# First q and k by tiles, and the order of splits, clears and copies around it, in a one-core attention and mixture-of-experts kernel

## The reference

```
attention: q, k, v are (4, 8, 576, 64); window of 64 keys back, causal
    scores = q k^T / 8, masked; softmax; times v  -> x (2304, 512)
mixture of experts, E = 8, F = 1024:
    noisy = x @ w_gate + log1p(exp(x @ w_noise)) * noise
    the two largest of noisy per row choose two experts, softmax of the two gives their weights
    out[row] += weight * (relu(x[row] @ w1[e]) @ w2[e])
dense part, F2 = 2048:
    h = x @ w_in;  g = h * clip(h + 3, 0, 6) / 6;  out = g @ w_out
```

## Time and profile before

| | |
|---|---|
| median of 3 runs | 1018.13 us (1018.12 to 1018.77) |
| profiled execution, its own time | 1019.22 us |
| its span, first to last instruction | 1017.5 us |
| TensorE busy | 988.1 us, 97% |
| VectorE, ScalarE, GpSimd busy | 417.8, 227.7, 423.5 us |
| mean granted TensorE clock | 0.991 |

### The profile page before, as it was taken

The page is one execution under the profiler, slowest core; times in us unless marked ns, Lnnn a source line. Parts: engine busy times, 40 slices in busy tenths (PEclk is TensorE's granted clock), DMA queues, the critical chain, the costliest instruction groups (busy, mean ns, idle before and its releaser), DMA issues.

```text
span 1017.5 us, 18019 instructions
## 1 busy us (share of the span) xinstructions
PE 988.1 (97%) x7108; PEld 877.5 (86%) x7108; DVE 417.8 (41%) x897; ACT 227.7 (22%) x537; POOL 423.5 (42%) x326
## 2 busy tenths in 40 slices
PE   7989889999999999999999999999999999999998
PEld 6777668989889898989989989999999999999997
DVE  3578764313222222213222255545445445355333
ACT  4666521111111111111111121111111211111111
POOL 3067976993855739192855729101101001000000
PEclk9999879999999999999999999999999999999999
DMA  9699876764452716263342433200101111000000
GB/s 181 128 207 247 271 258 222 246 186 150 135 185 90 230 61 208 70 180 122 125 145 86 151 106 125 64 32 21 42 31 41 41 31 41 31 1 1 32 1 31
DMA packets 125878, 115.94 MB, mean 114 GB/s; under 512 B 64912, under 2 KB 93520, under 8 KB 125808
## 3 DMA queue, kind: packets, MB, share of 16 engines
q1 hardware_dynamic: 106368, 75.36, 27.0%
q10 hardware_dynamic: 13680, 20.75, 6.0%
q0 software_dynamic: 5760, 18.88, 5.8%
HBM read 75.90 MB, written 39.06 MB: 113 GB/s over the span
## 4 chain that ended last, share of the span: by engine, by line
PE 81%; SPq 7%; POOL 5%; DMA 3%; issue 2%; DVE 1%; ACT 0%; ACTq 0%; POOLq 0%; DVEq 0%
PE PS L1635 20%; PE PS L1755 20%; PE PS L1739 19%; PE PS L1618 19%; SPq L500 3%; SPq L490 3%; POOL x_sorted L711 3%; PE PS L1602 1%; POOL W L690 1%; POOL W L680 1%; PE PS L1680 1%; DMA x_sorted<-zeros 1%; DMA y_sorted<-y_sb 0%; PE PS L1498 0%; DMA stage<-in_moe_w_dram 0%
## 5 line engine op out<-in xcount | busy, mean ns | idle before, releaser
L1635 PE MATMUL PS<-W,hs_room 128*128 128x512 f32 (+1 forms) x960 | 245.2, 399 | 0.1
L1618 PEld LDWEIGHTS PS<-xs,W 128*128 128x128 f32 x1536 | 231.0, 189 | 10.8 <-issue 0.2
L1618 PE MATMUL PS<-xs,W 128*128 128x256 f32 (+2 forms) x1536 | 239.7, 307 | 0.0
L1755 PE MATMUL PS<-W,gs 128*128 128x512 f32 x864 | 217.0, 396 | 0.9 <-DVE gs L1353 0.9
L1739 PE MATMUL PS<-x2s,W 128*128 128x384 f32 x1152 | 216.6, 337 | 0.0
L1739 PEld LDWEIGHTS PS<-x2s,W 128*128 128x128 f32 x1152 | 201.4, 188 | 7.2
L680 POOL TENSOR_TENSOR W<-stage,ones_f 128x1024 fp32r<-128x1024 f32 (+1 forms) x100 | 147.6, 1484 | 136.5 <-PE PS L1635 133.1
L1635 PEld LDWEIGHTS PS<-W,hs_room 128*128 128x128 f32 (+1 forms) x960 | 172.3, 186 | 34.6 <-DVE hs_room L1203 0.3
L1755 PEld LDWEIGHTS PS<-W,gs 128*128 128x128 f32 x864 | 161.5, 188 | 31.5 <-issue 1.6
L690 POOL TENSOR_TENSOR W<-stage,W 128x1024 fp32r<-128x1024 f32 (+1 forms) x100 | 185.4, 1863 | 5.8
L1203 DVE SCALAR_TENSOR_TENSOR hs_room<-PS,hs_room 128x256 fp32r<-128x256 f32 (+2 forms) x128 | 61.9, 484 | 290.6 <-ACT hs_room L899 290.6
(11 more groups left out here) (133 smaller groups left out, 574.4 us busy)
## 6 DMA issues: line engine op xcount, KB each, us to landing
stage<-in_moe_w_dram SPq DMA_DIRECT2D x64, 512.0 KB, 4.2
x_sorted<-zeros SPq DMA_DIRECT2D x7, 1280.0 KB, 7.6
y_sorted<-y_sb ACTq DMA_DIRECT2D x33, 256.0 KB, 3.7
x_in<-x_sorted ACTq DMA_DIRECT2D x31, 256.0 KB, 4.3
vD<-in_v_dram SPq DMA_DIRECT2D x72, 64.0 KB, 2.8
out_dram<-o_sb SPq DMA_DIRECT2D x18, 256.0 KB, 2.1
stage<-in_moe_w_in_dram SPq DMA_DIRECT2D x8, 512.0 KB, 3.9
stage<-in_moe_w_out_dram SPq DMA_DIRECT2D x8, 512.0 KB, 3.8
```

Of the source, the lines that this page charges most:

```text
L1618: last = nc.tensor.matmul(HP_[:, c % 2, 0:n], W[:, par, 0, b, at:at + P], xs[part][:, a, kd, 0:n], start=start, stop=(kd == KD - 1 and (a, ...
L1635: last = nc.tensor.matmul(Y[0:n, first + t, :], hs[:, c % 2, a, t * P:t * P + n], W[:, par, 1, b, c * DM:(c + 1) * DM], start=(c == 0 and ...
L1755: last = nc.tensor.matmul(OP[:, tt, :], gs[:, c % 2, a, tt * P:(tt + 1) * P], W[:, 1, c // FC, b, at:at + DM], start=(c == 0 and (a, b) == ...
```

## The change

- Start. Item 0 is now tile 0 with all heads and item 1 tile 1 with all heads (`turn_tile`), so `scores(0)` runs before the transposes of tile 1. `transpose_p(0, 0)` comes before item 2, and item 2 is turned into two other PSUM banks, so it does not wait for `exps(0)`. v of tile 0 goes through ScalarE's queue, the gate weights through GpSimd's, v of tile 1 is issued before chunk 3.
- Chunks 4 and 8, which cross no batch, are loaded by four transfers and not six; `sem_inc` stands in for the missing counts.
- In iterations 5, 6, 7, 9, 10, 11, 13 and 14, at which a lot is routed, ScalarE copies k too (`move_both`, `chooses`).
- GpSimd no longer splits chunks 3 and 4 at tiles 12 and 13. Lots 0 and 1 are sent a little denser, chunk 3 is split between the eight transfers of lot 2, and chunks 4 and 5 after them. Chunks 6 and 7 are split by ScalarE (`beside_hi`) and VectorE (`beside_lo`) during expert 0.
- Weight chunk 7 is loaded at tile 17 and not 15, and three parts of `y_sorted` are cleared right behind it, where before one was cleared at 17 and two after the rows of expert 0 were there.
- The last lot is ranked behind `project` of chunk 1 and not behind `hidden` of chunk 3; `tables` and `places_in_y` come a chunk later.

```diff
-    FIRST_AT = (4, 6, 8, 10, 12, 13, 14, 15)
-    SPLIT_AT = (7, 8, 11, 12, 13)
+    FIRST_AT = (4, 6, 8, 10, 12, 13, 14, 17)
+    SPLIT_AT = (7, 8, 11)
+    BESIDE = 2
...
-    ZERO_AT = (16, 17)
+    ZERO_AT = (16, 17, 17, 17)
...
-    SCATTER_AT = {8: 0, 9: 1, 10: 2, 12: 3, 13: 4, 14: 5, 15: 6}
+    SCATTER_AT = {8: (0,), 9: (1,), 10: (2,), 12: (3,), 13: (4, 5), 14: (6,)}
...
-                if c and c % 2 == 0 and r == (crossed or [0])[0]:
+                if r in crossed(c):
...
+        def item_bank(n, side):
+            return PS[:, 5 + side, :] if n == 2 else SC[:, item_buf(n), side, :]
...
+        def chooses(T):
+            return any(due(T, after) for after in (3, 4, RANKS_AFTER))
...
             load_qk(1, both)
             load_qk(2, both)
-            load_v(0)
+            load_v(1)
             load_qk(3, both)
-            load_v(1)
-            for n, w in enumerate((wg, wn)):
-                sp.dma_start(wgn[:, :, n * E:(n + 1) * E], w.rearrange("(k p) e -> p k e", p=P)).then_inc(s_small, 16)
...
-                if T in ZERO_AT:
-                    zero_y(ZERO_AT.index(T))
+                for n in range(ZERO_PARTS):
+                    if ZERO_AT[n] == T:
+                        zero_y(n)
...
-            load_expert(1, 0, QCH)
-            for n in range(len(ZERO_AT), ZERO_PARTS):
-                zero_y(n)
+            load_expert(1, 0, QCH - BESIDE)
...
             c = len(SPLIT_AT)
             first_there(c)
-            for n in range(2 * PIECES):
+            for n in range(2 * LOTS[FIRST_LOT][1]):
+                scatter(LOTS[FIRST_LOT][0] + n // 2, n % 2)
                 if n < PIECES:
                     split_hi(0, c, PIECES, n, n + 1)
                 else:
                     split_lo(0, c, c + 1, PIECES, n - PIECES, n - PIECES + 1)
-                scatter(LOTS[FIRST_LOT][0] + n // 2, n % 2)
-            for c in range(len(SPLIT_AT) + 1, SCH):
+                if n % 4 == 3:
+                    keep_x(kept)
+                    kept += 1
...
+            pool.sem_inc(w_half, BESIDE)
...
+            load_v_block(act, 0, 0)
             move_first(0)
+            load_v_block(act, 0, 1)
             move_first(1)
             exps(0)
+            move_pt(0, 0)
             move_first(2)
...
+                    if chooses(T):
+                        move_both(item_at(T))
+                    else:
+                        move_first(item_at(T))
...
+            def beside_hi(c):
+                act.wait_ge(stage_full[c % STAGES], 16 * (c // STAGES + 1))
...
+                nc.scalar.copy(W[:, 0, 1, 0, at], stage[:, c % STAGES, :]).then_inc(beside_half, 1)
...
+                    if first and c in (2, 3):
+                        beside_hi(SCH - BESIDE + c - 2)
...
-                if item_at(T) is not None:
+                if item_at(T) is not None and not chooses(T):
                     move_second(item_at(T))
...
+            def beside_lo(c):
...
+                dve.wait_ge(w_ready, c)
+                dve.wait_ge(beside_half, c - (SCH - BESIDE) + 1)
+                nc.vector.tensor_tensor(W[:, 0, 1, 1, at], stage[:, c % STAGES, :], W[:, 0, 1, 0, at].bitcast(F32),
+                                        ALU.subtract).then_inc(w_ready, 1)
...
-            turn_qk(0)
-            turn_qk(1)
+            turn_tile(0)
             scores(0)
+            turn_tile(1)
             scores(1)
+            transpose_p(0, 0)
             turn_qk(2)
-            transpose_p(0, 0)
...
-                        if first and part == 0 and c == 3:
-                            rank(NB - 1, TILES)
...
                         project(e, par, part, c - 1)
+                        if first and part == 0 and c == 2:
+                            rank(NB - 1, TILES)
```

More of the change, by code:

```diff
@@ L376, in half, with crossed @@
             return divmod(2 * T + s, KB)
+        def crossed(c):
+            return [r for r in range(TK) if half(c * TK + r, 0)[0] != half(c * TK + r, 1)[0]]
         def pieces(c):
-            crossed = [r for r in range(TK) if half(c * TK + r, 0)[0] != half(c * TK + r, 1)[0]]
-            assert len(crossed) <= 1 and not (crossed and c % 2)
+            assert len(crossed(c)) <= 1 and not (crossed(c) and c % 2)
             for r in range(TK):
-                if c and c % 2 == 0 and r == (crossed or [0])[0]:
+                if r in crossed(c):
                     for s in range(2):
@@ L472, in unit, with load_v_block @@
             return 2 * FC * e + FC * part + c
+        def load_v_block(eng, t, s):
+            b, i = half(t, s)
+            for x in range(2):
+                eng.dma_start(vD[WIN * x:WIN * (x + 1), t % RV, s, :, 0:D],
+                              v[b].rearrange("(h x) r d -> x r h d", x=2)[x, i * WIN:(i + 1) * WIN])\
+                    .then_inc(v_full[t % RV], 16)
         w1_c = w1.rearrange("e (c p) f -> (e c) p f", p=P)
@@ L492, in load_qk @@
                             .then_inc(raw_full[raw_slot(c)], 16)
+                if c % 2 == 0 and not crossed(c):
+                    sp.sem_inc(raw_full[raw_slot(c)], 32)
             def load_v(t):
@@ L735, in _ @@
                 keep_x(T - 2)
-                if T in SCATTER_AT:
-                    scatter(SCATTER_AT[T], 0)
+                transfers = [(t, k) for t in SCATTER_AT.get(T, ()) for k in range(2)]
+                if transfers:
+                    scatter(*transfers[0])
                 if T in SPLIT_AT:
@@ L754, in _ @@
                     split_lo(0, c, c + 1, PIECES, n - PIECES, n - PIECES + 1)
-                scatter(LOTS[FIRST_LOT][0] + n // 2, n % 2)
-            for c in range(len(SPLIT_AT) + 1, SCH):
+                if n % 4 == 3:
+                    keep_x(kept)
+                    kept += 1
+            keep_x(kept)
+            kept += 1
+            for c in range(len(SPLIT_AT) + 1, SCH - BESIDE):
                 first_there(c)
@@ L759, in _ @@
                 split_lo(0, c, c + 1, PIECES)
-                if c == len(SPLIT_AT) + 1:
-                    for t in range(max(SCATTER_AT) - 1, TILES - 1):
-                        keep_x(t)
-            keep_x(TILES - 1)
+                keep_x(kept)
+                kept += 1
+            assert kept == TILES
+            pool.sem_inc(w_half, BESIDE)
             for t in range(LOTS[FIRST_LOT + 1][0], TILES):
@@ L1284, in expert @@
                 for c in range(FC):
+                    if first and c == 3:
+                        route(NB - 1, 5)
+                        nc.vector.tensor_copy(pad_row[:], base_e[0:1, :]).then_inc(pads_ready, 1)
+                        route(NB - 1, 6)
                     h_lo(e, 0, c)
@@ L1292, in expert @@
                             route(NB - 1, part)
-                    if first and c == 3:
-                        route(NB - 1, 5)
-                        nc.vector.tensor_copy(pad_row[:], base_e[0:1, :]).then_inc(pads_ready, 1)
-                        route(NB - 1, 6)
                     if first and c == 4:
+                        for n in range(SCH - BESIDE, SCH):
+                            beside_lo(n)
+                    if first and c == 5:
                         tables()
                         dve.wait_ge(tabs_ready, 1)
-                    if first and c == 5:
+                    if first and c == 6:
                         places_in_y()
```

79 lines of the change are left out of this document (43 added, 36 removed).

## The result

| | before | changed |
|---|---|---|
| median of 16 runs each, taken together | 1018.52 us (1016.9 to 1022.25) | 1022.38 us (1021.22 to 1026.25) |
| profiled execution | 1019.22 us | 1021.22 us |
| its span | 1017.5 us | 1019.3 us |
| first `hidden` of expert 0 | 139.65 us | 136.48 us |
| from there to the end | 877.85 us | 882.8 us |

The ratio is 1.0039 (95% interval 1.0029 to 1.0049): **slower by 0.4%**, where 1015.0 us, 0.3% faster, was forecast. On another chip the ratio was 1.0024 (1.0012 to 1.0036). The last two rows of the table hold the case: in these two traces the attention gave 3.17 us, the 3.1 of the forecast, and 4.95 us went behind it, in a place priced at 0.

A forecast was written before the change was run, and what follows sets the result against it. The attention ahead of expert 0's first `hidden` was taken as the only place to win. Terms 2.2 + 1.3 + 0 + 1.2 + 1.4 + 0 - 3.0 = 3.1 us off 1018.13 gave 1015.0 us, range 1010.5 to 1018.5.

The forecast's parts named there:

- In expert 0, price 0: Expert 0: the added chunk splits by ScalarE and VectorE fit TensorE's slots of 4.1 us, so they cost 0.
- Ranking the last lot a chunk sooner is off the path: Expert 0: earlier ranking of the last lot doesn't matter, since its rows are needed some 15 us later.
- Any wait in expert 0 for `h_split`: Expert 0: a TensorE wait for the split of `hidden`, listed beforehand as showing the prediction wrong.
- First tiles, 2.2 us: Kernel start: earlier first scores win 1.6 us, v of tile 1 ahead of chunk 3 wins 0.6; bounds -0.9 to 4.2.
- rival 2: Start: the DMA engines own it, so the first two terms are 0.6 us each; 1017.3 us, chance 0.15.
- SP's queue, 1.3 us: Attention loads: fewer SP issues bring chunk 4 3.5 us sooner, its stall shrinks from 1.64 to 0.3; gain 0 to 1.64.
- chunk 5, 0: Attention: TensorE and SP's queue both 3.5 us ahead, so the stall at chunk 5 stays; gain 0 (0 to 2.0).
- k by ScalarE, 1.2 us: Eight routing iterations: VectorE loses a 0.68 us copy, shortening TensorE's waits; gain 1.2 us (0 to 2.0).
- Splits away, 1.4 us: Tiles 12 and 13: without GpSimd splits the wait for `chosen_b` in lot 2's routing goes; gain 1.4 us (0.7 to 1.9).
- Clears, 3.0 lost: End of attention: clears issued just ahead of expert 0's row loads delay them; 3.0 us lost (0 to 7.4).
- `hidden` near 136.5: End of attention: expert 0's first `hidden` expected near 136.5 us, with a span of 878 us behind it as before.
- Rival 3: End of attention: loads queue behind clears in full, 7.4 us, last transfer held 2.0 more; slower, 1021.4 us, chance 0.08.

The follow-up runs named there:

- run 7: Changed kernel, but GpSimd starts expert 1's split only after VectorE's `h_lo` of chunk 7: 1018.13 us, 0.9981 of before.
- run 9: Kernel before, with only `places_in_y` and the last lot's gates moved from behind chunk 5 to behind chunk 6: 1.0095 of before.
- run 11: First half of the change alone, but v of tile 0 issued by SP behind q and k of chunk 2: 0.9984 of before.
- 8: First half of the change alone (start, q and k transfers, v(0), gate weights, k by ScalarE); splits, lots, clears, ranks as before: 0.9972 of before.
- 10: First half of the change alone, without ScalarE's copies of k: 0.9971 of before.
- 5: The changed kernel unaltered, profiled again on a second chip beside the kernel before: 1.0024 of before.
- number 13: Changed kernel with expert 1's split held back, clears at tiles 14 and 15, two behind loads of expert 1's first chunks: 0.9962 and 0.9976 of before.

## Why the prediction was wrong

**In expert 0, price 0: here it fell.** The steps that failed are "TensorE is the cover; price 0" and "Ranking the last lot a chunk sooner is off the path". I asked whether VectorE's two new subtractions fit into a slot (they do, 2.47 us for both) and what GpSimd might do to them, but not what the earlier ranking sets going. The split of expert 1 came sooner and the same change put nine small instructions later, into it. I had the rule of the lock in hand and used it at iteration 14 alone. The runs showed 4.9 us in place of 0: a wait of 2.78 us for `h_lo`, slower groups behind it, and 3.17 - 4.95 = -1.8 us of span between the two traces. That the profile says so is a reading; that one wait takes 4.9 us off (run 7) and that the places moved by a chunk put 9 us on the old kernel (run 9) shows it. "Any wait in expert 0 for `h_split`" was among my own signs of being wrong, and it is this one.

**First tiles, 2.2 us: failed.** The first scores came at 7.46 (near 8 forecast), but tile 3's scores 1.4 us later than before, below my lower bound of -0.9. "A stall at chunk 2 over 1 us" was named as a sign of being wrong; it was 2.53. Two causes. v(0) ahead of chunk 2 costs it 1.4 us (run 11); I had 1.5 for it, but only in the lower bound. And what the first scores win turns into a wait for chunk 2, behind which TensorE runs at half rate and loses 1.6 us: the step held no price for a wait that merely moves. So far this is rival 2, which had 0.15; its other half, that SP's queue gains only 0.6, did not come.

**SP's queue, 1.3 us, and chunk 5, 0: right sum by luck, wrong parts.** The 3.5 us that the queue was to run ahead are 4.7 - 2.7 + 1.5, and no row gives the last 1.5; without it the queue is 2.0 us ahead, and the stall at chunk 4 does not shrink. In the first profile both stalls are gone, 3.6 us, and tile 9's scores come 3.5 us sooner (60.87 against 64.34), which is my 2.2 + 1.3. Since the start gave nothing, the queue gave more. On the second chip part of chunk 5's stall stays (0.73 us) and the gain there is 1.6 us (62.71 against 64.31).

**k by ScalarE, 1.2 us: not shown.** Iteration 11 is 0.78 us shorter, the total the same with and without it (runs 8 and 10).

**Splits away, 1.4 us: right.** The rank of lot 2 waits for nothing, and the last transfer begins at 124.05 and 124.47 in 5 and 7 against 125.85 in 8: 1.4 to 1.8 us.

**Clears, 3.0 lost: right** in size, 2.5 to 3.0 from issue to turn (5.2 to 5.8 against 2.7). That one clear does it alone was not foreseen. The estimate of 2.6 us by the packets' turns in the Trainium skill (DMA: Bandwidth & Descriptors, Queues, rings and completion order) fits these numbers as well as the row of the slowed transfer did.

**`hidden` near 136.5, so 3.1 us for the attention: met** in the first profile (136.48), by luck. Its parts were wrong both ways, and the medians speak for about 1 us; on the second chip the traces have 138.45 and 138.01 against 139.49, 1.0 and 1.5 us. So some 2 us of the 7.4 between 1015.0 and 1022.38 are missing here, nearly 5 in expert 0, and 0.4 is the kernel before, which took 1018.52 in 16 runs and not 1018.13.

Rival 3 had the sign and nearly the time (1021.4) by another mechanism, the clears in full, which is not what happened.

A version that beats both is number 13: 0.9962 and 0.9976 of before, 2.4 to 3.9 us, and 5 to 8 less than the changed kernel. The first half alone has 0.9972, inside the intervals of both, so that the second half wins anything is not shown.

## What to carry to other kernels

When a change makes an engine finish sooner, follow what it starts next, and lay that against what other engines do at that time: here GpSimd's split began 2.4 us sooner, counted from the first `hidden`, and met a chain of small VectorE instructions that the same change had moved 4.4 us later. Small instructions are the worst neighbours of long ones that lock them out: each can lose most of a long instruction, so their duration alone (0.8 us) says nothing of their price (6.2 us). Cover that is counted in one slot of TensorE must be held against the chain with its waits, and an engine with time to spare can be worth holding back: one wait won 4.9 us here. And look at where a profiled execution lies among its runs before its stages are taken as typical: here it hid some 2 us, by the estimate above.
